# Where TensorE turns the gathered rows of the tile after next in the expert stage of a three-stage kernel

## The reference

```python
logits = x @ w_gate + modality_bias[modality_id]
e_idx = argmax(logits); gate_w = softmax(logits)[e_idx]
h = np.maximum(x[mask] @ w1[e], 0.0)            # 512 -> 1024
out[mask] = gate_w[mask, None] * (h @ w2[e])    # 1024 -> 512
```

## Time and profile before

| | |
|---|---|
| median of 3 runs | 923.59 us (923.16 to 925.59) |
| profiled execution, its own time | 922.83 us |
| its span, first to last instruction | 921.1 us |
| TensorE products busy | 852.1 us, 93% |
| DVE, ACT, POOL busy | 506.0, 429.7, 210.7 us |
| mean granted clock of TensorE | 0.972 |

### The profile page before, as it was taken

The page is one execution under the profiler, slowest core; times in us unless marked ns, Lnnn a source line. Parts: engine busy times, 40 slices in busy tenths (PEclk is TensorE's granted clock), DMA queues, the critical chain, the costliest instruction groups (busy, mean ns, idle before and its releaser), DMA issues.

```text
span 921.1 us, 16050 instructions
## 1 busy us (share of the span) xinstructions
PE 852.1 (93%) x4845; PEld 727.6 (79%) x4846; DVE 506.0 (55%) x1039; ACT 429.7 (47%) x1186; POOL 210.7 (23%) x202
## 2 busy tenths in 40 slices
PE   5787888888999999999999999999699999999994
PEld 3566666667998998998988998998578888888883
DVE  6999999963665565555555555568762111111110
ACT  3777767773555345445445445466053222222221
POOL 2566767643121001001001002000311111111110
PEclk9999999987999999999999999999899999999998
DMA  5555555320100000000000000212060111111110
GB/s 114 145 150 141 146 141 144 95 56 25 47 23 35 1 1 35 0 0 10 24 0 0 34 0 0 90 60 69 35 229 35 46 46 37 42 46 46 38 42 13
DMA packets 88197, 51.57 MB, mean 56 GB/s; under 512 B 64480, under 2 KB 77280, under 8 KB 88160
## 3 DMA queue, kind: packets, MB, share of 16 engines
q1 hardware_dynamic: 85040, 41.16, 16.0%
q0 software_dynamic: 3120, 9.96, 3.2%
HBM read 41.67 MB, written 9.70 MB: 56 GB/s over the span
## 4 chain that ended last, share of the span: by engine, by line
PE 77%; DVE 13%; issue 4%; ACT 2%; SPq 1%; POOL 1%; DVEq 1%; DMA 0%; ACTq 0%; POOLq 0%
PE ps L1443 8%; PE ps L1445 8%; PE ps L1444 8%; PE ps L1333 7%; PE ps L1334 7%; PE ps L1335 7%; PE ps L1309 7%; PE ps L1308 7%; PE ps L1314 7%; DVE ssum L895 3%; DVE smax L885 3%; DVE kdz L870 2%; PE ps L1234 2%; PE ps L1466 2%; PE ps L1350 1%
## 5 line engine op out<-in xcount | busy, mean ns | idle before, releaser
L729 ACT ACTIVATE Eb<-ps 128x384 f32<-128x384 f32 x96 | 47.2, 492 | 145.9 <-PE ps L1314 145.7
L992 DVE TENSOR_SCALAR Tb<-Eb 128x384 f32<-128x384 f32 x96 | 35.4, 369 | 131.1 <-ACT Eb L729 131.1
L659 ACT ACTIVATE prob<-ps,nmax 96x111 f32<-96x111 f32 (+1 forms) x256 | 87.8, 356 | 26.5 <-DVE nmax L889 26.3
L1309 PE MATMUL ps<-xh,WA 128*128 128x384 f32 x288 | 98.5, 342 | 0.0
L1308 PE MATMUL ps<-xh,WA 128*128 128x384 f32 x288 | 97.8, 340 | 0.0
L562 POOL TENSOR_TENSOR xl<-xT,xh 128x384 fp32r<-128x384 f32 x24 | 26.8, 1145 | 280.3 <-ACT xh L701 280.3
L1333 PE MATMUL ps<-WA,gh 128*128 128x512 f32 x216 | 86.8, 402 | 0.2 <-DVE gl L943 0.2
L1335 PE MATMUL ps<-WA,gl 128*128 128x512 f32 x216 | 85.4, 395 | 0.0
L1334 PE MATMUL ps<-WA,gh 128*128 128x512 f32 x216 | 85.2, 394 | 0.0
L738 ACT ACTIVATE Rb<-Tb 128x384 f32<-128x384 f32 x96 | 50.4, 525 | 60.8 <-DVE Tb L994 60.8
L1174 DVE TENSOR_TENSOR hTl<-ps,hTh 128x1024 fp32r<-128x1024 f32 x19 | 23.3, 1224 | 97.6 <-ACT hTh L792 97.6
(11 more groups left out here) (218 smaller groups left out, 2009.1 us busy)
## 6 DMA issues: line engine op xcount, KB each, us to landing
wsraw<-in_moe_w_dram SPq DMA_DIRECT2D x32, 256.0 KB, 3.3
vwin<-in_v_dram SPq DMA_DIRECT2D x32, 166.5 KB
qraw<-in_q_dram SPq DMA_DIRECT2D x32, 144.0 KB, 3.0
kraw<-in_k_dram SPq DMA_DIRECT2D x32, 144.0 KB, 3.1
vdraw<-in_v_dram SPq DMA_DIRECT2D x32, 144.0 KB
y_rows<-yrow SPq DMA_DIRECT2D x6, 768.0 KB, 3.6
wraw<-in_moe_w_in_dram SPq DMA_DIRECT2D x12, 256.0 KB, 5.6
wraw<-in_moe_w_out_dram SPq DMA_DIRECT2D x12, 256.0 KB, 3.4
```

The source lines that it names most:

```text
L659: last = act.activation(prob[0:np_, a.s6, n * w:(n + 1) * w], ps[0:np_, o:o + w], ACT.Exp, scale=sc, bias=nmax[0:np_, a.s6, n:n + 1], accu ...
L1309: pe.matmul(dst, lo, xh[:, kk, :], start=False, stop=False)
```

## The change

In the loop, `turn_x` moves behind `turn_h` and takes the tile t + 2 instead of t + 1. The code ahead of the loop shrinks: tile 1 is now done by the loop, which begins at 1, and `turn_x(2)` stands directly behind `turn_h(0)`, ahead of `experts_in(1)`. Since the last turn of the loop now turns tile `n_tiles` + 1, POOL gathers one tile more, and the tables have one column more.

```diff
-        NSX = NSLOT + 1
+        NSX = NSLOT + 2
@@ POOL
-                if t <= NTOK:
+                if t <= NTOK + 1:
                     gather(t)
-                elif t <= NSLOT:
-                    with pool.If(n_tiles > t - 1):
+                elif t <= NSLOT + 1:
+                    with pool.If(n_tiles > t - 2):
                         gather(t)
@@ TensorE
             turn_x(1)
             turn_h(0)
-            experts_in(1)
             turn_x(2)
-            experts_out(0)
-            turn_h(1)
-            with pe.Fori(2, n_tiles) as t:
+            with pe.Fori(1, n_tiles) as t:
                 experts_in(t)
-                turn_x(t + 1)
                 experts_out(t - 1)
                 turn_h(t)
+                turn_x(t + 2)
```

## The result

The changed kernel takes 926.68 us in the median of 14 runs (924.57 to 930.59), against 923.35 us of the kernel before in 14 runs beside it (921.98 to 925.59). The ratio is 1.0038 (95% interval 1.0028 to 1.0049), that is 3.5 us more. The profiled execution has a span of 925.0 us, 3.9 more than before.

What follows compares the result with a forecast made beforehand. It took TensorE as the bound, busy 93% of the span. Terms −0.2 + 2.7 + 0.2 + 0.15 + 1.0 = +3.9 us gave 926.7 from the profiled run or 927.5 from the median; it said 927.1, range 924.6 to 929.8.

Steps and rivals of the forecast that it cites:

- The steady loop: Expert loop: joining transpose groups of 4 and 8 into 12 saves 0.01 us in each of 18 turns, 0.2 us.
- The wait for the gather: Loop start: TensorE stands before turn_x(2) until about 682.8 us for tile 2's rows, gather 3.3 us, upper end 5.1.
- The reads behind it: Loop start, behind the gather wait: two table reads delay products in(1) by 1.53 us, plus 0.2 for loop entry.
- The smaller parts: Outside the steady loop: wider tables +0.2 us, one more test at the end +0.15, extra gather and turn 0.
- The clock: Loop start, 678.60 to about 684.5 us: TensorE's clock falls to its lower level, costing 1.0 us, bounds 0 and 1.8.
- The sum: Whole kernel: all terms together make it 3.9 us slower, forecast 927.1 us, chance 0.50.
- Rival 1: Loop start: the clock stays up, all else as forecast; +2.9 us, 926.1; chance 0.22.
- Rival 2: Loop start: the queue reads both numbers while transposes wait for rows; +1.7 us in all, about 925; chance 0.12.
- Rival 3: Steady loop: a switch between products and transposes costs 0.09 us or more; at 0.09 net +1.4 us; chance 0.10.
- Rival 4: Loop's turn: table reads lose cover, 0 to 1.52 us per tile; at 0.38, 6.8 us, so 934; chance 0.06.

Runs made afterwards that it cites:

- e8_reads_and_warm: Changed kernel with tile 1 written out, 8 unused products behind turn_h(0), then tile 1's two table reads, then turn_x(2); ratio to the kernel before 0.9997.
- e2_start_only: Kernel before with one line moved, turn_x(2) ahead of products in(1); loop, tables and gathers as before; ratio to the kernel before 1.0038.
- e6_old_order_filled: Kernel before with tile 1's two table reads ahead of turn_h(0) and 9 unused products ahead of the last tile's products; ratio to the kernel before 0.9984.
- e7_split_turn: Kernel before with the loop's four transposes of x spread, one ahead of each of the first four slabs of products out; ratio to the kernel before 1.0003.
- e4_reads_early: Changed kernel with tile 1 written out and its two table reads ahead of turn_x(2); the loop begins at 2; ratio to the kernel before 1.0028.
- e1_loop_only: Changed kernel with its start undone: products in(1) ahead of turn_x(2) again, tile 1 written out, new order kept in the loop; ratio to the kernel before 1.0007.
- e5_own_buffer: Changed kernel with a separate buffer for tile 2's gathered rows, whose gather waits for nothing; ratio to the kernel before 1.0005.
- e3_warm_in_wait: Changed kernel with 8 unused products between turn_h(0) and turn_x(2); ratio to the kernel before 1.0038.

## Why the prediction was right, step by step

- **The steady loop.** Gain 0.2 us said, 0.24 measured, and the cost of a switch (0.01 us from the chain) came out at 0.014 to 0.016. Scatter and gather are 1.33 us apart on POOL now, as said to be "nearly together", and no gather was waited for in the loop.
- **The wait for the gather.** It ended 4.35 us after turn_x(1) began (682.09 against 677.74); 682.8 − 678.6 = 4.2 was said. The transfer took 3.4 us instead of 3.3. In e8_reads_and_warm it took 4.8: the upper end kept for it (5.1) was nearly reached once in the five profiled executions that waited for it.
- **The reads behind it.** 1.53 + 0.2 us said, 1.92 measured: 1.67 for transposes and reads, 0.25 for the loop's entry. (682.8 + 1.53 + 0.2 is 684.53 and not 684.55; nothing hangs on it.) Together with the wait, the start of the loop cost 3.47 − 0.44 = 3.0 us, where 2.7 was said.
- **The smaller parts.** The tables took less than the 0.2 us said: the three selections on POOL grew from 5.14 to 5.23 us. Behind the last product the kernel lost 0.29 us (0.04 and 0.25), where one test had been put at 0.15. (The working has 4.9 us left for the tests before; from the end of the issue, 921.1 − 914.57 − 2.8 leaves 3.7. The 0.15 doesn't hang on it.) The extra turn at the end cost nothing.
- **The clock.** The fall came, and this term was sized too small: 1.0 us said, 1.65 measured. The low stretch began almost with the products (684.4 and 684.01), so hardly any of it lay over waiting. The upper bound of 1.8 held.
- **The sum.** +3.9 us was said. The profiled executions give 3.03 + 1.61 (19.00 − 6.27 less the 11.12 that 24 products in and 24 out take in the kernel before) − 0.24 + 0.36 = 4.76. The median moved by 3.3 us and the ratio says 3.5, less than that. Part of that is the choice of executions: the profiled one of before took 922.83 us, 0.5 below the median of its kernel, and that of after 927.0, 0.3 above. The clock of the last tile is no part of it, since both had the full one there (5.39 and 5.46 us; 6.96 in e2_start_only with the same end). Among the 14 runs of the changed kernel time and mean clock go together (correlation −0.9; the fastest, 924.57 us, had 0.969 and the slowest, 930.59 us, 0.958), but elsewhere the link is weak: −0.4 in 30 and −0.2 in 35 runs of the kernel before, none in e6_old_order_filled and e7_split_turn. So the clock is one source of the spread and the rest is open. How many of the 1.65 us of the start belong to the median run was not separated.
- **Luck.** The mechanism is what the runs show. That 927.1 us came within 0.4 us of the 926.68 measured is luck in part: the start was sized 0.3 us and the clock 0.65 us too small, and the median moved by 1.4 us less than the starts in the profiles.

**Rivals.** Rival 1 (the clock stays up) didn't hold in the profiled execution; e8_reads_and_warm, where it did stay up, shows what that is worth. Rival 2 (the queue reads its numbers while the transposes still wait) is refuted by the row of 1.49 us "issue" and by e4_reads_early. Rival 3 (dear switches) is refuted by e7_split_turn. Rival 4 (the reads at the loop's turn come out of cover) didn't happen in the changed kernel. It did happen once in e1_loop_only, at the entry (0.90 us idle, 1.15 in the loop's length against the changed kernel), where a split was late, and small gaps of the first turn stand in e5_own_buffer (12.59 us instead of 12.32) and e6_old_order_filled too.

## What to carry to other kernels

Before a step is moved ahead of another one, look at what the step waits for at its first use, not in the steady loop: with one buffer, a gather that is hidden behind 24 products in each turn is open in the turn where the products stand behind it. A wait that stops an engine's queue costs also what the queue has to do behind it (here two table reads: 1.67 us from the transposes to the products, 0.42 with the reads ahead of the wait), so reads belong ahead of waits. And an idle stretch on TensorE is priced with the products behind it: here 1.65 us on top of 3.0.

## What was not expected of the hardware

- The clock fell after the last wait of 2.0 to 2.5 us in six of nine executions, and not in the other three. The same work ahead of it went both ways: before against e2_start_only, after against e3_warm_in_wait. One execution that shows 1.00 at a place, as the earlier trace rows for 900 to 906.1, doesn't say that the next will.
- Products put into the idle stretch kept the clock up in one execution (e8_reads_and_warm) and not in another (e3_warm_in_wait), with nearly the same idle time left behind them, 1.49 and 1.68 us. The runs don't say what made the difference.
- e8_reads_and_warm, whose turn_h(1) is 2.9 us later than that of before in its profile, was not slower in the timed runs (0.9997, at most 1.0005). e5_own_buffer (1.4 us later, 1.0005) is at the edge of what its interval allows, 1.0015. A profiled execution places an effect well, but single ones differ by more than 3 us ahead of the change and by 1.5 us at the last tile. So an effect of this size needs both, its place from the profile and its size from many timed runs.
